# Halving the instructions that make the low parts of the second-layer weights, for all experts

## The chip, the cores and the metric

The kernel runs on one core of a Trainium2 chip. The metric is the device time of one execution in microseconds (us), lower being better. Engines are named as in the profile: PE is TensorE, DVE VectorE, ACT ScalarE, POOL GpSimd and SP SyncE.

## The reference

Three layers follow one another. Attention over a window of 128 positions gives x, 2304 rows of 512. Eight experts then share the rows: each takes the 288 rows that it likes best among those not yet taken, and sends them through two matrices. A dense layer of two matrices with a sigmoid gate ends it.

```python
def _moe_ref(x, w_gate, w1, w2):            # x (2304, 512), w1 (8, 512, 1024), w2 (8, 1024, 512)
    ...                                     # assigned[token] = expert, 288 tokens each, by sorted logits
    for e in range(E):
        mask = assigned == e
        h = np.maximum(x[mask] @ w1[e], 0.0)
        out[mask] = h @ w2[e]

def _moe2_ref(x, w_in, w_out):              # w_in (512, 2048), w_out (2048, 512)
    h = x @ w_in
    g = h * (1.0 / (1.0 + np.exp(-h)))
    return g @ w_out
```

## The kernel before, in words

The first 160 us or so are the attention, which also keeps the dense layer's weights in SBUF (res_h, res_l). Then the experts run in the order in which a ranking on the core names them, and each is followed by its share of the dense layer. STAGES lists the 16 stages: "A" is an expert's two layers, "M" the dense layer for a batch of rows (256, 256, 256 and 384, twice).

Each product is made of three: a value is kept as a high part, rounded to the matmul's input type, and a low part, the remainder. `product` multiplies high by high, high by low, low by high. For the experts' weights this splitting is done while the kernel runs. A tile of the first layer (wa) or of the second (wb) is 128x512. SP loads wb_raw (L1089), ACT rounds it to wb_h (L1385), and POOL subtracts, wb_l = wb_raw - wb_h, in `low_b` (L1156). wb_l lies over wb_raw. For wa the last step is DVE's, in `low_a` (L1647). Both rings have four tiles. Tile w belongs to expert w // 8, and f = w % 8.

An A stage runs the products a (first layer, f = 0 to 7, 12 matmuls each) and b (second layer, 12 matmuls each) in the order a0 a1 a2 b0 a3 b1 ... a7 b5 b6 b7. An M stage runs 16 of each in the same order. SLOTS is this list; every engine walks it, does its own part of each slot, and waits on semaphores for the others. SPLIT_B says in which slot a tile of wb is split: tiles 0 to 3 of an expert near the end of the M stage before it, one to each a slot; tile f from 4 on in slot b of f - 2.

In M stages POOL also makes the low part of the hidden values, h_l (L1168), issues the gather of the next expert's rows (L1130) and the scatter of finished ones (L1144). In A stages DVE makes h_l (L1712).

DVE and PE rank the tokens for the next expert meanwhile, in short steps at fixed slots (HOOK_AT). DVE compares all keys with 91 thresholds (`test`, L1492, 128x1820), PE counts them in 20 small matmuls (L1192), DVE finds what was reached (L1516), PE sums it (L1196), DVE updates `base` (L1521) and starts the next test. PE's steps stand in order between the products: in an A stage step 0 follows b2, step 1 follows a5, step 2 follows b4, step 3 follows a7 and step 4 follows b7. DVE's part after step 3 is a test. Expert 7's A stage has no such steps.

PE waits for wb_l once ahead of each product b (L1279, in `expert_b`), not once for each half. In the first expert, w < FT1 = 8, `low_b` has two instructions of 256 columns to each tile.

Of the kernel before, what the change touches and what calls it, by code (L numbers as in the profile page):

```python
# [16 lines left out]
DM = H * D  # L17
# [9 lines left out]
FT1, FT2 = F1 // P, F2 // P  # L27
# [903 lines left out]
def experts(nc, w1, w2, x_dram, out, keep):  # L931
# [4 lines left out]
    with ExitStack() as ctx:  # L936
# [6 lines left out]
        def sem(name):  # L943
            return ctx.enter_context(nc.semaphore(name))
# [84 lines left out]
        wb_high, wb_low = sem("wb_high"), sem("wb_low")  # L1029
# [20 lines left out]
        def h_cols(s, f):  # L1050

            width = CAP if STAGES[s][0] == "A" else BATCH[STAGES[s][1]][1]
            return slice(COLS * (f % 3), COLS * (f % 3) + width)
# [15 lines left out]
        @block.sync  # L1069
        def _(sp):  # L1070
            expert = []
            for kind, w in LOADS:
                j, f = divmod(w, FT1)
                if j == len(expert):
                    sp.wait_ge(id_known, j + 1)
                    expert.append(sp.value_load(ids[0:1, j:j + 1], min_val=0, max_val=E - 1))
                e = expert[j]
                if (kind, w) == LOADS[4]:
                    sp.wait_ge(fetch_sent, 1)
                if kind == "a":  # L1080
                    if w >= RING:
                        sp.wait_ge(a_done, A_NO[tile_stage(w - RING)])
                    sp.dma_start(wa_raw[w % RING][:].rearrange("p (c m) -> p c m", c=DC),
                                 w1[bass.ds(e, 1), :, P * f:P * (f + 1)].rearrange("o (c p) m -> p (o c) m", p=P)
                                 ).then_inc(wa_loaded[w % RING], 16)
                else:
                    if w >= RING:
                        sp.wait_ge(b_done, B_NO[tile_stage(w - RING)])
                    sp.dma_start(wb_raw[w % RING][:],  # L1089
                                 w2[bass.ds(e, 1), P * f:P * (f + 1), :].rearrange("o p m -> (o p) m")  # L1090
                                 ).then_inc(wb_loaded[w % RING], 16)
            sp.wait_ge(scattered, 16 * TILES_OUT[-1])

        @block.gpsimd
        def _(pool):
            pool.memset(ones[:], 1.0).then_inc(ones_ready, 1)

            def thresholds(j):

                for n, step in enumerate(STEPS[j][0:HIGH_ROUNDS]):  # L1100
                    pool.iota(rungs[j][:, n, :], pattern=[[step, KW[j]]], base=0, channel_multiplier=0,
                              allow_small_or_imprecise_dtypes=True).then_inc(rungs_ready, 1)

            thresholds(0)
            pool.memset(test[:, KW[0] * AHEAD:SECOND], 0.0).then_inc(rungs_ready, 1)
            pool.memset(test[:, SECOND + KW[0] * (NT - AHEAD):SECOND + KW[0] * (NT - AHEAD - 1) + P], 0.0
                        ).then_inc(rungs_ready, 1)
            pool.iota(iota_row[:], pattern=[[1, BLOCK]], base=0, channel_multiplier=0,
                      allow_small_or_imprecise_dtypes=True).then_inc(init_seq, 1)
            pool.iota(part_no[:], pattern=[[0, 1]], base=0, channel_multiplier=1,  # L1110
                      allow_small_or_imprecise_dtypes=True).then_inc(init_seq, 1)

            pool.iota(tile_base[:].rearrange("p (b t) -> p b t", b=B), pattern=[[S // 64, B], [P // 64, TB]], base=0,
                      channel_multiplier=0, allow_small_or_imprecise_dtypes=True).then_inc(init_seq, 1)
            pool.wait_ge(ones_ready, 1)
            pool.affine_select(out=before[:], in_=ones[:], compare_op=ALU.is_gt, fill=0.0, base=0,
                               pattern=[[1, P]], channel_multiplier=-1).then_inc(init_done, 1)
            thresholds(1)
            pool.memset(test[:, KW[1] * NT:KW[1] * (NT - 1) + P], 0.0).then_inc(rungs_ready, 1)

            def fetch(j):

                pool.wait_ge(tokens_known, GR * (j + 1))
                if j >= 1:
                    pool.wait_ge(xt_done, DC * j)
                else:
                    for stored in keep["x_stored"]:
                        pool.wait_ge(stored, 2 * 16 * B)
                for a in range(GR):
                    pool.indirect_dma_start(  # L1130
                        out=rows[:, a, :], out_offset=None, in_=x_dram,
                        in_offset=bass.IndirectOffsetOnAxis(ap=tokens[:, GR * j + a:GR * j + a + 1], axis=0)
                    ).then_inc(gathered[a], 16)

            def store(k):

                pool.wait_ge(out_known, k + 1)
                for t in range(BATCH[k][1] // P):
                    if t % 2 == 0:
                        pool.wait_ge(out_even, EVEN_OUT[k] + t // 2 + 1)  # L1140
                    else:
                        pool.wait_ge(out_odd, ODD_OUT[k] + t // 2 + 1)
                    n = TILES_OUT[k] + t
                    pool.indirect_dma_start(  # L1144
                        out=out, in_=out_rows[t], in_offset=None,
                        out_offset=bass.IndirectOffsetOnAxis(ap=out_tokens[:, n:n + 1], axis=0)
                    ).then_inc(scattered, 16)

            def low_b(w):

                pool.wait_ge(wb_high, w + 1)

                n = 2 if w < FT1 else 1
                for piece in range(n):
                    at = slice(DM // n * piece, DM // n * (piece + 1))
                    pool.tensor_tensor(wb_l[w % RING][:, at], wb_raw[w % RING][:, at], wb_h[w % RING][:, at].bitcast(FP32),  # L1156
                                       ALU.subtract).then_inc(wb_low, 1)

            fetch(0)
            pool.memset(mark[:], 0.0).then_inc(fetch_sent, 1)  # L1160
            for n, (s, kind, f) in enumerate(SLOTS):
                if n in STORE_AT:
                    store(STORE_AT[n])
                if kind == "a" and STAGES[s][0] == "M" and (s, f) != (len(STAGES) - 1, FT2 - 1):
                    g = FT2 * STAGES[s][1] + f
                    cols = h_cols(s, f)
                    pool.wait_ge(g_high, g + 1)
                    pool.tensor_tensor(h_l[:, cols], h_raw[:, cols], h_h[:, cols].bitcast(FP32), ALU.subtract  # L1168
                                       ).then_inc(g_low, 1)
                for w in SPLIT_B.get(n, []):  # L1170
                    low_b(w)
                if n in FETCH_AT:
                    fetch(FETCH_AT[n])
            store(len(BATCH) - 1)

        @block.tensor
        def _(pe):
# [60 lines left out]
            def product(out_, weights_h, weights_l, cols_h, cols_l, start, stop):  # L1238

                nc.tensor.matmul(out_, weights_h, cols_h, start=start, stop=False)  # L1240
                nc.tensor.matmul(out_, weights_h, cols_l, start=False, stop=False)  # L1241
                return nc.tensor.matmul(out_, weights_l, cols_h, start=False, stop=stop)  # L1242
# [32 lines left out]
            def expert_b(s, i, f):  # L1275

                w = FT1 * i + f
                pe.wait_ge(relu_low, w + 1)
                pe.wait_ge(wb_low, w + 1 + min(w + 1, FT1))  # L1279
                if f == 0 and i >= 1:  # L1280
                    pe.wait_ge(out_even, EVEN_OUT[i])
                    pe.wait_ge(out_odd, ODD_OUT[i])
                for c in range(DC):
                    m = slice(P * c, P * (c + 1))
                    last = product(acc[c][:, 0:CAP], wb_h[w % RING][:, m], wb_l[w % RING][:, m],
                                   h_h[:, h_cols(s, f)], h_l[:, h_cols(s, f)], f == 0, f == FT1 - 1)
                    if f == FT1 - 1 and c < DC - 1:
                        last.then_inc(acc_done, 1)
                last.then_inc(b_done, 1)
# [465 lines left out]
```

## Time and profile before

| | |
|---|---|
| median of 3 runs | 849.39 us (848.35 to 851.86) |
| profiled execution, its own time | 851.72 us |
| its span | 849.7 us |
| PE busy | 823.1 us, 97% |
| DVE busy | 485.2 us, 57% |
| ACT busy | 331.4 us, 39% |
| POOL busy | 305.5 us, 36% |
| wb_l on POOL (L1156) | 72 instructions, 87.2 us |

A busy time is the sum over an engine's instructions, overlaps counted once. The span is shorter than the execution's own time by what lies ahead of the first and behind the last instruction. In the timeline a row has an instruction's start and duration in us, engine, line, operation, what it writes and reads, and in brackets the idle time before it and what ended that.

### The profile page before, as it was taken

The page shows a single profiled execution, that of the slowest core. Times are in us where ns is not written, and L with a number is a line of the kernel's source. Part 1 is how long each engine was busy: PE and PEld are TensorE (multiplying, and loading weights), DVE is VectorE, ACT ScalarE, POOL GpSimd, SP SyncE. Part 2 cuts the span into 40 slices and gives each one's busy share as a digit, 9 for nine tenths or more (in the row PEclk, how much of TensorE's full clock was granted, in tenths as well). Part 3 has the DMA queues.
Part 4 walks back from the last instruction along what each step waited for, and adds up shares of the span by engine and source line. Part 5 has one row for each costly group of instructions (what it writes and reads, how often), then busy time and mean ns, then how long its engine had stood idle before and what let it go on. Part 6 is the DMA issues. An engine that isn't in the chain of part 4 may idle for free.

```text
span 849.7 us, 17963 instructions
## 1 busy us (share of the span) xinstructions
PE 823.1 (97%) x6903; PEld 746.8 (88%) x6903; DVE 485.2 (57%) x1562; ACT 331.4 (39%) x767; POOL 305.5 (36%) x343
## 2 busy tenths in 40 slices
PE   9999999649999999999999999999999999999997
PEld 7888888539989998998899889988998999899996
DVE  6778777666654756566565343846665475542111
ACT  4666666304224333432433224333332433343221
POOL 1013447714336234333622244234323623433222
PEclk9999999858999999999999999999999999999999
DMA  9789987324022304300340031204302230430000
GB/s 132 128 179 197 175 177 211 102 84 130 14 74 65 114 1 128 101 26 14 115 125 2 8 120 59 78 2 128 113 14 68 71 115 1 128 99 26 1 1 37
DMA packets 149764, 71.43 MB, mean 84 GB/s; under 512 B 98736, under 2 KB 136112, under 8 KB 149680
## 3 DMA queue, kind: packets, MB, share of 16 engines
q1 hardware_dynamic: 144336, 60.56, 28.7%
q0 software_dynamic: 2976, 9.44, 3.5%
q8 instruction: 55, 0.90, 0.5%
q10 hardware_dynamic: 2368, 0.30, 0.3%
q14 instruction: 29, 0.24, 0.1%
HBM read 60.83 MB, written 9.44 MB: 83 GB/s over the span
## 4 chain that ended last, share of the span: by engine, by line
PE 73%; DVE 4%; DMA 1%; issue 1%; POOL 1%; ACT 0%; SPq 0%; POOLq 0%; DVEq 0%; ACTq 0%
PE hp L1240 12%; PE hp L1241 11%; PE hp L1242 11%; PE acc L1325 8%; PE acc L1327 8%; PE acc L1326 8%; PE acc L1240 4%; PE acc L1242 3%; PE acc L1241 3%; PE rt L1192 2%; DVE wa_l L1647 1%; DMA wa_raw<-in_moe_w_dram 1%; DVE test L1492 1%; DMA x_rows_sb<-x_rows,tokens 1%; PE rt L1207 1%
## 5 line engine op out<-in xcount | busy, mean ns | idle before, releaser
L1168 POOL TENSOR_TENSOR h_l<-h_raw,h_h 128x256 fp32r<-128x256 f32 (+1 forms) x127 | 114.7, 903 | 260.8 <-ACT h_h L1449 260.7
L1718 DVE TENSOR_TENSOR h_raw<-hp,gate 128x256 f32<-128x256 f32 (+1 forms) x128 | 58.5, 457 | 179.7 <-ACT gate L1441 178.2
L1240 PE MATMUL hp<-xy_h,res_h 128*128 128x256 f32 (+1 forms) x512 | 154.0, 301 | 0.0
L1241 PE MATMUL hp<-xy_l,res_h 128*128 128x256 f32 (+1 forms) x512 | 151.4, 296 | 0.0
L1242 PE MATMUL hp<-xy_h,res_l 128*128 128x256 f32 (+1 forms) x512 | 151.2, 295 | 0.0
L1156 POOL TENSOR_TENSOR wb_l<-wb_raw,wb_h 128x512 fp32r<-128x512 f32 (+1 forms) x72 | 87.2, 1216 | 129.0 <-ACT wb_h L1385 129.0
L1441 ACT ACTIVATE gate<-hp 128x256 f32<-128x256 f32 (+1 forms) x128 | 52.7, 412 | 195.4 <-PE hp L1242 181.0
L1325 PE MATMUL acc<-res_h,h_h 128*128 128x512 f32 x288 | 116.6, 405 | 0.0
L1327 PE MATMUL acc<-res_h,h_l 128*128 128x512 f32 x288 | 113.6, 394 | 0.0
L1326 PE MATMUL acc<-res_l,h_h 128*128 128x512 f32 x288 | 113.5, 394 | 0.0
L1240 PEld LDWEIGHTS hp<-xy_h,res_h 128*128 128x128 f32 x512 | 96.5, 188 | 3.6
L1241 PEld LDWEIGHTS hp<-xy_l,res_h 128*128 128x128 f32 x512 | 96.4, 188 | 3.4
L1242 PEld LDWEIGHTS hp<-xy_h,res_l 128*128 128x128 f32 x512 | 96.5, 188 | 0.0
L1449 ACT ACTIVATE h_h<-h_raw 128x256 fp32r<-128x256 f32 (+1 forms) x128 | 56.6, 442 | 68.9 <-DVE h_raw L1718 68.9
L1240 PE MATMUL acc<-h_h,wb_h 128*128 128x288 f32 x256 | 76.5, 299 | 0.0
L1240 PE MATMUL hp<-xy_h,wa_h 128*128 128x288 f32 x252 | 75.6, 300 | 0.0
L1242 PE MATMUL acc<-h_h,wb_l 128*128 128x288 f32 x256 | 75.2, 294 | 0.0
L1241 PE MATMUL acc<-h_l,wb_h 128*128 128x288 f32 x256 | 75.2, 294 | 0.0
L1241 PE MATMUL hp<-xy_l,wa_h 128*128 128x288 f32 x252 | 74.5, 296 | 0.0
L1242 PE MATMUL hp<-xy_h,wa_l 128*128 128x288 f32 x252 | 74.4, 295 | 0.0
L537 PE MATMUL o_ps<-v_rows,pT 128*128 128x65 f32 x576 | 71.5, 269 | 0.0
L537 PEld LDWEIGHTS o_ps<-v_rows,pT 128*128 128x128 f32 x576 | 69.4, 192 | 0.0
(236 smaller groups left out, 1679.7 us busy)
## 6 DMA issues: line engine op xcount, KB each, us to landing
wa_raw<-in_moe_w_dram SPq DMA_DIRECT2D x64, 256.0 KB, 3.4
wb_raw<-in_moe_w_dram SPq DMA_DIRECT2D x64, 256.0 KB
k_rows<-in_k_dram SPq DMA_DIRECT2D x64, 72.0 KB, 3.4
q_rows<-in_q_dram SPq DMA_DIRECT2D x60, 72.0 KB, 2.5
v_rows<-in_v_dram SPq DMA_DIRECT2D x32, 128.0 KB, 4.3
x_rows<-x_rows_sb SPq DMA_DIRECT2D x8, 512.0 KB, 3.3
stage<-in_moe_w_in_dram SPq DMA_DIRECT2D x8, 512.0 KB, 4.7
stage<-in_moe_w_out_dram SPq DMA_DIRECT2D x8, 512.0 KB, 3.7
```

What stands on the lines that cost most here:

```text
L537: last = nc.tensor.matmul(o_ps[s % 2][:, o:o + D + 1], weights, v_rows[g % RING_IN][:, kt, h, :], start=(i == 0), stop=(i == len(blocks) - 1))
L1156: pool.tensor_tensor(wb_l[w % RING][:, at], wb_raw[w % RING][:, at], wb_h[w % RING][:, at].bitcast(FP32), ALU.subtract).then_inc(wb_low, 1)
L1168: pool.tensor_tensor(h_l[:, cols], h_raw[:, cols], h_h[:, cols].bitcast(FP32), ALU.subtract).then_inc(g_low, 1)
L1240: nc.tensor.matmul(out_, weights_h, cols_h, start=start, stop=False)
L1241: nc.tensor.matmul(out_, weights_h, cols_l, start=False, stop=False)
L1242: return nc.tensor.matmul(out_, weights_l, cols_h, start=False, stop=stop)
L1325: nc.tensor.matmul(acc[t][:], h_h[:, m], res_h[:, o:o + DM], start=(b == 0), stop=False)
L1326: nc.tensor.matmul(acc[t][:], h_h[:, m], res_l[:, o:o + DM], start=False, stop=False)
L1327: last = nc.tensor.matmul(acc[t][:], h_l[:, m], res_h[:, o:o + DM], start=False, stop=(b == FT2 - 1))
L1441: nc.scalar.activation(gate[:, 0:width], hp[(A_NO[s, f] - 1) % 2][:, 0:width], ACT.Sigmoid).then_inc(sig_done, 1)
L1449: nc.scalar.activation(h_h[:, h_cols(s, f)], h_raw[:, h_cols(s, f)], ACT.Copy).then_inc(g_high, 1)
L1718: nc.vector.tensor_tensor(h_raw[:, h_cols(s, f)], hp[(A_NO[s, f] - 1) % 2][:, 0:width], gate[:, 0:width], ALU.mult).then_inc(g_done, 1)
```

## The change

`low_b` now makes two instructions of 256 columns for every tile, each of which raises the semaphore wb_low by one, and `expert_b` waits for twice the number of tiles. Nothing else is touched.

```diff
                 pool.wait_ge(wb_high, w + 1)
 
-                n = 2 if w < FT1 else 1
-                for piece in range(n):
-                    at = slice(DM // n * piece, DM // n * (piece + 1))
+                for piece in range(2):
+                    at = slice(DM // 2 * piece, DM // 2 * (piece + 1))
                     pool.tensor_tensor(wb_l[w % RING][:, at], wb_raw[w % RING][:, at], wb_h[w % RING][:, at].bitcast(FP32),
                                        ALU.subtract).then_inc(wb_low, 1)
...
                 pe.wait_ge(relu_low, w + 1)
-                pe.wait_ge(wb_low, w + 1 + min(w + 1, FT1))
+                pe.wait_ge(wb_low, 2 * (w + 1))
```

## Rows read from the trace of the kernel before

**Rows 1.** The page: busy time of TensorE, and its granted clock in 40 slices.
```profile
PE 823.1 (97%) x6903; PEld 746.8 (88%) x6903; DVE 485.2 (57%) x1562; ACT 331.4 (39%) x767; POOL 305.5 (36%) x343
...
PEclk9999999858999999999999999999999999999999
```
**Rows 2.** All waits of TensorE, 285 to 845 us: total, times, longest.
```profile
PE rt L1196 <- DVE reached L1516: 0.9, 2, 0.8
```
**Rows 3.** Groups by form: the whole-tile instructions (count, busy, mean ns, idle before).
```profile
L1156 POOL TENSOR_TENSOR wb_l<-wb_raw,wb_h 128x512 fp32r<-128x512 f32 x56 | 73.2, 1307 | 111.6 <-ACT wb_h L1385 111.6
```
**Rows 4.** Timeline, halves and DVE in the first expert; last row: L61 alone.
```profile
198.04 1.43 POOL L1156 TENSOR_TENSOR wb_l<-wb_raw,wb_h 128x256 fp32r<-128x256 f32 x2 [8.75 <-ACT wb_h L1385]
...
205.43 0.73 POOL L1156 TENSOR_TENSOR wb_l<-wb_raw,wb_h 128x256 fp32r<-128x256 f32 x1 [0.53 <-ACT wb_h L1385]
205.46 0.88 DVE L61 TENSOR_TENSOR liked<-liked,best 128x160 f32<-128x160 f32 x1
206.12 0.82 POOL L1156 TENSOR_TENSOR wb_l<-wb_raw,wb_h 128x256 fp32r<-128x256 f32 x1
...
208.25 2.11 DVE L1492 SCALAR_TENSOR_TENSOR test<-rungs,base,key_hi 128x1820 bf16<-128x1820 f32 x1
208.59 2.37 POOL L1156 TENSOR_TENSOR wb_l<-wb_raw,wb_h 128x256 fp32r<-128x256 f32 x1 [1.65 <-ACT wb_h L1385]
210.28 1.22 DVE L1647 TENSOR_TENSOR wa_l<-wa_raw,wa_h 128x512 fp32r<-128x512 f32 x1
210.91 1.19 POOL L1156 TENSOR_TENSOR wb_l<-wb_raw,wb_h 128x256 fp32r<-128x256 f32 x1
...
357.17 0.32 DVE L61 TENSOR_TENSOR liked<-liked,best 128x160 f32<-128x160 f32 x1
```
**Rows 5.** Timeline, expert 1: tiles 5 and 7, the last test, products b5 and b7.
```profile
289.10 1.32 POOL L1156 TENSOR_TENSOR wb_l<-wb_raw,wb_h 128x512 fp32r<-128x512 f32 x1 [1.97 <-ACT wb_h L1385]
...
295.03 0.38 PE L1240 MATMUL acc<-h_h,wb_h 128*128 128x288 f32 x1
...
296.19 1.33 POOL L1156 TENSOR_TENSOR wb_l<-wb_raw,wb_h 128x512 fp32r<-128x512 f32 x1 [2.50 <-ACT wb_h L1385]
296.39 3.04 DVE L1492 SCALAR_TENSOR_TENSOR test<-rungs,base,key_hi 128x1820 bf16<-128x1820 f32 x1
298.28 0.29 PE L1240 MATMUL acc<-h_h,wb_h 128*128 128x288 f32 x1
```
**Rows 6.** Timeline, expert 6: tile 7 and the start of b7.
```profile
699.72 1.32 POOL L1156 TENSOR_TENSOR wb_l<-wb_raw,wb_h 128x512 fp32r<-128x512 f32 x1 [2.48 <-ACT wb_h L1385]
...
701.80 0.29 PE L1240 MATMUL acc<-h_h,wb_h 128*128 128x288 f32 x1
```
**Rows 7.** Timeline, expert 7: tile 7 and the start of b7.
```profile
774.71 1.30 POOL L1156 TENSOR_TENSOR wb_l<-wb_raw,wb_h 128x512 fp32r<-128x512 f32 x1 [1.90 <-ACT wb_h L1385]
776.66 0.29 PE L1240 MATMUL acc<-h_h,wb_h 128*128 128x288 f32 x1
```
**Rows 8.** Timeline, the end of the first M stage: a tile and the next h_l.
```profile
262.01 1.30 POOL L1156 TENSOR_TENSOR wb_l<-wb_raw,wb_h 128x512 fp32r<-128x512 f32 x1
264.06 0.73 POOL L1168 TENSOR_TENSOR h_l<-h_raw,h_h 128x256 fp32r<-128x256 f32 x1 [0.75 <-ACT h_h L1449]
```
**Rows 9.** Timeline: expert 2 ahead of TensorE's wait, and its two waits.
```profile
361.83 1.28 POOL L1156 TENSOR_TENSOR wb_l<-wb_raw,wb_h 128x512 fp32r<-128x512 f32 x1 [9.65 <-ACT wb_h L1385]
361.87 1.79 DVE L1647 TENSOR_TENSOR wa_l<-wa_raw,wa_h 128x512 fp32r<-128x512 f32 x1
...
364.75 0.18 PE L1196 MATMUL rt<-reached,ones 128*128 128x8 bf16 x1 [0.76 <-DVE reached L1516]
...
539.24 0.18 PE L1196 MATMUL rt<-reached,ones 128*128 128x8 bf16 x1 [0.16 <-DVE reached L1516]
```
**Rows 10.** Windows: stretch, busy time of PE, PEld, DVE, ACT, POOL, granted clock, DMA.
```profile
170.00:175.00 5.00, 1.79 (x42) 1.45 (x42) 3.38 (x14) 0.00 (x0) 0.00 (x0) 0.50 0.00 0
...
353.00:377.00 24.00, 23.24 (x216) 22.72 (x215) 18.08 (x34) 8.02 (x18) 5.17 (x4) 1.00 0.31 94
```

## The prediction

> **What bounds the kernel now.** I read the page's busy times first, then the waits, then the timeline of each engine in one expert after another. TensorE is busy 97% of the span at full granted clock from the experts on [rows 1], and between 285 and 845 us it waited for anything only twice, 0.9 us in all [rows 2]. So the kernel is one long row of TensorE instructions, and the change can cost or give time in two ways alone: by making TensorE wait where it doesn't now, or by removing one of those two waits. POOL has time to spare (36% busy), so the longer work on it counts for nothing as a sum; what counts is when a tile of wb_l is complete, and when VectorE (DVE) gets its turn beside POOL.
>
> **What is added.** 56 whole-tile instructions (experts 1 to 7, eight tiles each) of 1.31 us [rows 3] become 112 halves. A half alone takes 0.73 us, and a pair that nothing disturbs 1.43 us (the second is recorded from 0.69 us after the first and lasts 0.73) [rows 4], so each tile is 0.12 us later and POOL has 56 x 0.12 = 7 us more work, off the path. The first expert's pairs stay. TensorE's wait is now for twice the tile number, as many as POOL signals, so it releases at the second half of the same tile; it gains nothing from the first half, since its one wait stands ahead of the whole tile.
>
> **What the halves do to DVE's turn.** DVE and POOL exclude each other in some instructions. DVE's test, which compares 128x1820 values, takes 2.11 us alone [rows 4], but 3.04 us where it starts 0.20 us after a whole wb_l [rows 5]: it ends 1.91 us after POOL's instruction (299.43 against 297.52), as if it had waited for that one's end. The other way round, a half that POOL started at 208.59, inside a test that ended at 210.36, ended at 210.96, 0.60 us after the test [rows 4]. Who is next after a half, with a DVE instruction waiting and POOL's second half behind? The first expert shows it. The mask of `liked` (L61) started at 205.46, 0.03 us behind a half, and ended at 206.34; alone it takes 0.32. The second half, recorded from 206.12, ended at 206.94, which is 0.60 after L61's end. With POOL's second half first, L61 would have ended no earlier than 206.9. Likewise wa_l at 210.28 waited for the half that ended at 210.96 and ended at 211.50, and the next half, from 210.91, ended at 212.10, again 0.60 us behind [rows 4]. So DVE slips in between two halves. With a whole tile it can't.
>
> The Trainium skill, "SBUF — State Buffer", section "Who interferes with whom", says that a DVE instruction with two SBUF inputs and a GpSimd instruction that reads SBUF share a port pair as an exclusive lock held for the whole instruction. The 3.04 us agree. The same page gives about 115 ns from DVE's end to the blocked side's start for a transfer's descriptors; with a half of 0.73 behind it the second half would end 0.85 us after the test and the sum below would be 1.5 us higher, by that estimate. The measured 0.60 decides.
>
> **Where that meets TensorE.** Take the last tile (f = 7) of expert 1 [rows 5]. Now: wb_l starts at 296.19, is complete at 297.52, and TensorE starts its product (b of f = 7) at 298.28, without waiting: slack 0.76 us. DVE's test of the next ranking starts at 296.39. After the change, on the same clock: first half ends at 296.19 + 0.73 = 296.92; the test goes next and ends at 296.92 + 1.91 = 298.83; the second half ends at 298.83 + 0.60 = 299.43; a semaphore takes some 0.05 us to TensorE, so the product starts at 299.48 and not at 298.28. Stall: 1.20 us. Ahead of it TensorE has nothing else to do, since its stream is in order; behind it stands everything, the 20 small ranking products, the rest of the stage, the next.
>
> The order repeats, for both instructions hang on the same h_h of ScalarE: in experts 1 to 6 the last wb_l starts at 296.19, 373.07, 449.41, 547.54, 623.86 and 699.72, the test 0.19 or 0.20 us later, and the product 2.08 or 2.09 us after wb_l (the first is shown in [rows 5], the last in [rows 6]). Six stalls x 1.20 = 7.2 us.
>
> **Where it doesn't.** Tile f = 5 meets a test in five experts too (wb_l at 289.10 in expert 1), and would be complete at 289.10 + 0.73 + 1.91 + 0.60 = 292.34; its product starts at 295.03 [rows 5]: 2.7 us of cover, and if that were gone it would cost as much again as f = 7. In expert 2 it is only the one-column `base` that it meets. In expert 7 there is no ranking left: the last tile, 774.71 + 1.43 = 776.14, is still ahead of 776.66 [rows 7]. Tiles 0 to 3 are split in the dense stage behind a h_l; POOL is idle 0.75 us before the next h_l [rows 8], and a pair takes 0.12 more. Even with a DVE instruction between, the product that takes that h_l stands two products behind. Cost: 0; in the worst case 0.1 us x 28 = 3 us. SyncE's loads hang on TensorE's b_done and shift with it.
>
> **What is gained.** TensorE's two waits, 0.76 us at 364.75 and 0.16 us at 539.24, end at DVE's reached, which is late behind wa_l. In expert 2 wa_l started at 361.87, 0.04 us behind a whole wb_l, and took 1.79 us [rows 9]. By the first expert's pattern [rows 4] it takes 1.22, ending at 363.10 and not 363.66, and the second half ends at 363.10 + 0.60 = 363.70. The next wa_l, which would start at 363.39, waits for that and ends 0.54 later (as 211.50 stands to 210.96), at 364.24, not at 363.95 + 0.67 = 364.62: 0.4 us. In expert 4 the 0.16 us go whole. Sum of gains 0.56 us; bounds -0.9 (both waits vanish) and +0.3 (each wa_l sees 0.13 us more).
>
> **Sum.** 7.2 - 0.56 = +6.6 us: the profiled execution of 851.72 us (span 849.7 and 2.0 around it) would become 858.3. It was the high end of the three runs; from their median of 849.39 the same +6.6 gives 856.0. About 0.5%, 4.2 us, can be told from no change here; the forecast is 0.8%. Its own range: a stall of 0.9 to 1.5 us (each of the three terms, 0.73, 1.91 and 0.60, off by 0.1), gains 0 to 0.9: +4.5 to +9, so 853.9 to 858.4.
>
> **Rivals.** (A) POOL keeps the turn for its second half. Then the last tile is complete at P + 1.43, against the product at P + 2.09 (P: wb_l's start), so no stall, and DVE is 0.12 us later: the two waits grow to at most 1.2 us. Time 849.7. For it: halves are issued back to back in undisturbed pairs. Against it: the three places in [rows 4], all with DVE between; though none of these has a test waiting, only shorter instructions. Chance 0.14.
> (B) The other side: DVE's earlier turn is all that matters, because the second half still comes by P + 2.03. Place: the two waits of [rows 9]; price -0.9 us at most, plus run-to-run drift; it decides if a test between halves delays the second by less than 0.6 us instead of 2 us. That would need them to overlap, against the 2.37 us half of [rows 4]. Time 848.5. Chance 0.05.
> (C) The stalls do more: the granted clock falls after them. It stood at 0.50 (1.2 of 2.4 GHz) where TensorE was 36% busy [rows 10], but stayed at 1.00 through the 0.76 us wait of expert 2 [rows 10], and the new waits are 1.2 us. If half a microsecond more went after each, or the dense stage's 3 us came on top, it would be 859 to 861. Chance 0.06.
> Forecast: 0.75.
>
> The range of 849.0 to 860.0 holds the forecast, most of C and the upper part of A. Faster by over 0.5%: 0.02 (no mechanism reaches it, only drift on top of B); within 0.5%: 0.20 (A, the rest of B, and 0.03 from the weak end of the forecast); slower: 0.78 (the rest of the forecast and C).
>
> **What would show it.** In the waits, TensorE on wb_l of POOL: six times, about 1.2 us each, 7 us in all, in experts 1 to 6 and none in 7. In the timeline, the last tile's halves 0.73 us and about 2.5 us long, and the test between them 2.45 us, not 3.04. The clock stays at 1.00. The wait of expert 2 shrinks to about 0.4 us. Wrong, if the test ends after both halves (A), if the second half ends while the test runs (B), or if TensorE starts the last product within 0.2 us of where it does now.

## The result, and the profile after

| | before | after |
|---|---|---|
| median, 8 runs each | 849.62 us (847.55 to 854.01) | 855.74 us (855.21 to 858.5) |
| profiled execution, its own time | 851.72 us | 855.71 us |
| its span | 849.7 us | 853.8 us |

The changed kernel is slower: ratio 1.0074, 95% interval 1.0057 to 1.0091, so 6.3 us, between 4.8 and 7.7. Two executions at a lower granted clock are in no ratio: one of the kernel before (999.26 us, clock 0.746), timed beside the first four experiments, and one of their "A wait for each half" (900.66 us, 0.842). Each experiment's ratio is against the kernel before, timed beside it (medians 850.1, 849.87 and 849.61 us).

TensorE's waits from 285 us on (total, times, longest), against [rows 2]:

```profile
PE acc L1239 <- POOL wb_l L1155: 7.0, 6, 1.2
```

A wait that didn't exist before, six times, and the two waits for reached are gone. On the page POOL is busier and the clock is as before, against [rows 1]:

```profile
PE 822.1 (96%) x6903; PEld 744.5 (87%) x6903; DVE 478.8 (56%) x1562; ACT 331.4 (39%) x767; POOL 337.7 (40%) x399
...
PEclk9999999859999999999999999999999999999999
...
L1155 POOL TENSOR_TENSOR wb_l<-wb_raw,wb_h 128x256 fp32r<-128x256 f32 x128 | 119.3, 953 | 108.0 <-ACT wb_h L1384 107.9
```

POOL is busy 32 us longer, which is 25 us more than the 7 us that 56 instruction starts cost alone: the rest is halves that stand waiting for DVE, since a blocked instruction counts as busy. POOL's total says nothing of the cost; TensorE's waits do. Note also that DVE's busy time fell by 6 us, with the same instructions, in a slower kernel.

Now the last tile of expert 1, on POOL, DVE and TensorE, against [rows 5]. A timeline merges neighbours of one kind, so the pair appears as one row (x2), and its first half alone in a narrower window:

```profile
293.17 3.27 POOL L1155 TENSOR_TENSOR wb_l<-wb_raw,wb_h 128x256 fp32r<-128x256 f32 x2 [2.36 <-ACT wb_h L1384]
...
293.17 0.77 POOL L1155 TENSOR_TENSOR wb_l<-wb_raw,wb_h 128x256 fp32r<-128x256 f32 x1 [2.36 <-ACT wb_h L1384]
...
293.91 2.53 POOL L1155 TENSOR_TENSOR wb_l<-wb_raw,wb_h 128x256 fp32r<-128x256 f32 x1
...
293.37 2.48 DVE L1491 SCALAR_TENSOR_TENSOR test<-rungs,base,key_hi 128x1820 bf16<-128x1820 f32 x1
...
292.01 0.38 PE L1239 MATMUL acc<-h_h,wb_h 128*128 128x288 f32 x1
...
296.58 0.37 PE L1239 MATMUL acc<-h_h,wb_h 128*128 128x288 f32 x1 [1.17 <-POOL wb_l L1155]
```

The first half ends at 293.94, the test at 295.85 (1.91 later), the second half at 296.44 (0.58 to 0.59 later), the product b7 starts at 296.58 (0.15 later). Before, b7 started 3.25 us after b5 (295.03 to 298.28 in [rows 5]); now it is 4.57 us (292.01 to 296.58). So b7 starts 1.32 us late, 0.15 more than the 1.17 that the row calls idle: TensorE's matmuls overlap (one every 0.13 us, each recorded as 0.29 long), and the idle time is counted from the modelled end of the last one. Another 0.08 us goes behind the wait: b7's first matmul is recorded as 0.37 us long and the second starts at 296.79, 0.21 us after it, where before they started about 0.13 us apart (298.28 and 298.40). A stall costs 1.4 us in all. Expert 6 is the same, against [rows 6]:

```profile
702.37 3.27 POOL L1155 TENSOR_TENSOR wb_l<-wb_raw,wb_h 128x256 fp32r<-128x256 f32 x2 [2.33 <-ACT wb_h L1384]
702.57 2.48 DVE L1491 SCALAR_TENSOR_TENSOR test<-rungs,base,key_hi 128x1820 bf16<-128x1820 f32 x1
705.78 0.37 PE L1239 MATMUL acc<-h_h,wb_h 128*128 128x288 f32 x1 [1.17 <-POOL wb_l L1155]
```

In expert 7, where no test runs, the pair is undisturbed and b7, which begins at 780.74, doesn't wait, as in [rows 7]:

```profile
778.78 1.43 POOL L1155 TENSOR_TENSOR wb_l<-wb_raw,wb_h 128x256 fp32r<-128x256 f32 x2 [1.75 <-ACT wb_h L1384]
```

Where the time went, by the start of each expert's first product b (us from the span's start):

| expert | before | after | after minus before | growth over the expert ahead |
|---|---|---|---|---|
| 1 | 277.75 | 274.75 | -3.00 | |
| 2 | 353.75 | 352.14 | -1.61 | +1.39 |
| 3 | 430.98 | 429.76 | -1.22 | +0.39 |
| 4 | 528.84 | 529.02 | +0.18 | +1.40 |
| 5 | 605.44 | 606.65 | +1.21 | +1.03 |
| 6 | 681.39 | 684.04 | +2.65 | +1.44 |
| 7 | 757.61 | 761.68 | +4.07 | +1.42 |

Each row adds one stall of about 1.4 us, less in two of them where a wait of before went, and from expert 7 on nothing is added (92.09 us to the end of the span before, 92.12 after). The experts' part grew by 7.07 us. The profiled execution of before had come to them 3 us later than that of after: its first product of all started at 193.76 us with 1.76 us of waiting for gathered rows just before, against 192.71 us, and its granted clock was 0.95 between 195 and 226 us, against 1.00 (over its first 6.9 us of products 0.68, against 1.00 over the first 4.9 us after). The whole 3 us are there at the first expert's own first product b, 200.54 against 197.52 us. That is run-to-run drift ahead of the edited code, and it explains why the two spans differ by 4.1 us and not by 7.

### The profile page after: what moved, and what is told of

The parts are those of the page before. It is cut to its first block, busy times and chain, and to the rows that moved or that the text cites. A ratio compares the mean times of both kernels' runs of the same rounds, so it can differ in the third digit from the quotient of the medians.

```text
span 853.8 us, 18019 instructions
## 1 busy us (share of the span) xinstructions
PE 822.1 (96%) x6903; PEld 744.5 (87%) x6903; DVE 478.8 (56%) x1562; ACT 331.4 (39%) x767; POOL 337.7 (40%) x399
## 4 chain that ended last, share of the span: by engine, by line
PE 73%; POOL 3%; DVE 2%; ACT 1%; issue 1%; DMA 0%; POOLq 0%; DVEq 0%; ACTq 0%
PE hp L1239 12%; PE hp L1240 12%; PE hp L1241 12%; PE acc L1324 8%; PE acc L1326 8%; PE acc L1325 8%; PE acc L1239 3%; PE acc L1241 3%; PE acc L1240 3%; POOL wb_l L1155 2%; PE rt L1191 2%; PE rt L1206 0%; DVE test L1487 0%; PE acc L1233 0%; ACT wb_h L1384 0%
## 5 line engine op out<-in xcount | busy, mean ns | idle before, releaser
L1155 POOL TENSOR_TENSOR wb_l<-wb_raw,wb_h 128x256 fp32r<-128x256 f32 x128 | 119.3, 953 | 108.0 <-ACT wb_h L1384 107.9
```

## The experiments

Theory: a half lets DVE's test in ahead of the second half, which then waits for all of it, and the last tile of experts 1 to 6 has no slack for that. Each `PARTS[w]` below is the number of instructions for tile w, with TensorE's wait adapted to their sum.

**Only the last tile in halves.**

```diff
-                for piece in range(2):
+                for piece in range(PARTS[w]):
...
+PARTS = [2 if w < FT1 or w % FT1 == FT1 - 1 else 1 for w in range(E * FT1)]
```

> Halves only for the last tile (f = 7) of experts 1 to 7, and for the first expert as before; all other tiles whole. Theory (DVE's test slips in between the halves of the last tile): six waits of TensorE on wb_l of 1.16 us, so about +7 us against the kernel before, 856 to 857 us: all of the change's cost with 7 of its 56 added instructions. Rival (the 56 added instructions cost about evenly, as work of POOL or as delay of DVE in many places): 7 of 56 of 6 us, under +1 us.

Measured: 857.69 us, 0.7 above the range expected, ratio 1.0103 (1.0077 to 1.0129). Seven of the added instructions give the whole cost, and the rival's "under 1 us" is out. TensorE's waits from 275 to 785 us:

```profile
PE acc L1240 <- POOL wb_l L1156: 7.0, 6, 1.2
PE rt L1196 <- DVE reached L1516: 0.9, 1, 0.9
```

The new wait is the same; one wait for reached is back, in expert 2, whose tile 4 is whole here.

**All but the last tile in halves.**

```diff
+PARTS = [2 if w < FT1 or w % FT1 < FT1 - 1 else 1 for w in range(E * FT1)]
```

> Halves for all tiles but the last (f = 7) of experts 1 to 7, which stay whole: 49 of the 56 added instructions. Theory: no wait of TensorE on wb_l, within 1 us of the kernel before (849 to 850 us). Rival (added instructions cost evenly): +5 us.

Measured: 849.37 us, ratio 0.9986 (0.9972 to 1.0000). No wait on wb_l; one for reached of 0.34 us, in expert 5. The other 49 instructions, and the tests that split some of their tiles, cost nothing that can be measured.

**The test one slot later.**

```diff
-for _n in ((9, 10, 13, 14) if _j == 1 else (8, 9, 12, 13))
+for _n in ((9, 10, 13, 14) if _j == 1 else (8, 9, 12, 14))
```

> All tiles in halves, but step 3 of the ranking stands one slot later in experts 1 to 6 (behind b5 and not ahead of it), so DVE's test comes 1.6 us later, when the second half has started. Theory: the pair ends 1.43 us after its start, the test behind it at +3.3 us, and TensorE's waits on wb_l vanish; 849.5 to 850.5 us. Rival (the halves' later end alone, without the test, makes TensorE wait, or two signals cost): 855 to 856 us as with the change.

Measured: 848.82 us, ratio 0.9985 (0.9966 to 1.0005). Every tile is still in halves, and TensorE waits on none; it waits once for reached, 0.35 us in expert 5. POOL and DVE at the last tile of expert 1:

```profile
293.03 1.43 POOL L1155 TENSOR_TENSOR wb_l<-wb_raw,wb_h 128x256 fp32r<-128x256 f32 x2 [2.36 <-ACT wb_h L1384]
...
293.83 0.64 DVE L1520 SCALAR_TENSOR_TENSOR base<-digit,base 128x1 f32<-128x1 f32 x1
294.51 2.12 DVE L1491 SCALAR_TENSOR_TENSOR test<-rungs,base,key_hi 128x1820 bf16<-128x1820 f32 x1
```

Both run at their undisturbed length. `base`, one column wide, now meets the second half (0.64 us, not 0.16), and so holds the test back until POOL is done. So it is not the halves and not the second signal: it is the test between them.

**A wait for each half.**

```diff
-                pe.wait_ge(wb_low, 2 * (w + 1))
...
                 for c in range(DC):
+                    if c % 2 == 0:
+                        pe.wait_ge(wb_low, 2 * w + 1 + c // 2)
```

> All tiles in halves, and TensorE waits for the first half ahead of the product's first two column blocks and for the second half ahead of the third. Theory: b7 starts where it did before, runs 6 of its 12 matmuls (0.79 us) and then waits for the second half: 1.17 - 0.79 = 0.38 us six times, 2.3 us instead of 7.0, so 4.7 us less than the changed kernel, about 851 us. Rival (a wait ahead of the third block costs by itself, 64 times): no gain over the changed kernel, 855 us or more.

Measured: 852.72 us (852.61 without the execution at the lower clock), ratio 1.0031 (1.0014 to 1.0048), 3 us under the changed kernel's median, where 4.7 were expected. The wait moves behind six matmuls and shrinks from 1.17 to 0.30 us:

```profile
PE acc L1239 <- POOL wb_l L1155: 1.8, 6, 0.3
```

In the last tile of expert 1:

```profile
294.43 3.27 POOL L1155 TENSOR_TENSOR wb_l<-wb_raw,wb_h 128x256 fp32r<-128x256 f32 x2 [2.36 <-ACT wb_h L1385]
...
297.76 0.40 PE L1239 MATMUL acc<-h_h,wb_h 128*128 128x288 f32 x1 [0.30 <-POOL wb_l L1155]
```

I expected 0.38. The idle time reads low again: the matmul at 297.76 starts 0.59 us after the one ahead of it and the next 0.24 after that, both 0.13 undisturbed, so a stall costs 0.57 us. From expert 1's first product b to expert 7's the trace is 5.0 us shorter than the changed kernel's (481.89 against 486.93), which is six times the difference of 1.41 and 0.57; that the medians are only 3 us apart was not traced, but executions of one kernel spread by as much. The last tile's stall is a matter of when its second half is there.

**The test in two instructions.**

```diff
-                nc.vector.scalar_tensor_tensor(at_least, rung[:, None, :].to_broadcast([P, NT, k]),
+                for tiles in (slice(0, NT // 2), slice(NT // 2, NT)):
+                    last = nc.vector.scalar_tensor_tensor(at_least[:, tiles], ...
...
+                last.then_inc(dve_part, 1)
```

> The changed kernel, with DVE's test made by two instructions of 10 token tiles each, for experts 1 to 6's rankings (the wb_l tiles stay in halves). Theory (each side gets its turn when the other's instruction ends): POOL's second half waits for the first part of the test alone, about 0.95 us less, so TensorE's wait on wb_l falls from 1.17 to about 0.2 to 0.3 us six times; 850.5 to 852 us. Rival (once DVE has the turn it keeps it for all that it has queued): the waits stay at 1.2 us or grow by the second instruction's start, 856 to 857 us.

Measured: 851.96 us, ratio 1.0026 (1.0006 to 1.0047); six waits of 0.23 us on wb_l. They aren't all that this version pays: TensorE's wait for a test in the first expert is 0.86 us and not 0.24, and in expert 5 it waits 0.23 us for a h_l. In the last tile of expert 1:

```profile
293.37 2.33 POOL L1155 TENSOR_TENSOR wb_l<-wb_raw,wb_h 128x256 fp32r<-128x256 f32 x2 [2.36 <-ACT wb_h L1384]
...
293.56 1.53 DVE L1492 SCALAR_TENSOR_TENSOR test<-rungs,base,key_hi 128x910 bf16<-128x910 f32 x1
...
293.56 3.10 DVE L1492 SCALAR_TENSOR_TENSOR test<-rungs,base,key_hi 128x910 bf16<-128x910 f32 x2
```

First half to 294.14, first part of the test to 295.09, second half to 295.70 (0.6 behind it), second part of the test to 296.66 (0.96 behind that). The two engines take turns, instruction by instruction. The rival, DVE keeping the turn while it has more queued, is out.

**The last tile in four parts.**

```diff
+PARTS = [4 if w >= FT1 and w % FT1 == FT1 - 1 else 2 for w in range(E * FT1)]
```

> The last tile (f = 7) of experts 1 to 7 in four parts of 128 columns, all others in halves as in the changed kernel. Theory (one gap behind the first part lets the test in; after it nothing of DVE's is queued that excludes POOL): the first part ends some 0.3 us earlier and the test with it, but three parts come behind it and not one; in all two more instruction starts of 0.12 to 0.15 us, waits of 1.4 to 1.5 us, 857 to 858 us. Rival (a shorter first instruction shortens the wait, since the test starts earlier): waits under 1.0 us, 854 to 855 us.

Measured: 858.16 us, ratio 1.0095 (1.0065 to 1.0124); TensorE's waits from 275 to 785 us:

```profile
PE acc L1240 <- POOL wb_l L1156: 8.7, 6, 1.4
```

The timeline of the test and the tile in expert 1:

```profile
294.96 2.21 DVE L1492 SCALAR_TENSOR_TENSOR test<-rungs,base,key_hi 128x1820 bf16<-128x1820 f32 x1
...
294.76 3.54 POOL L1156 TENSOR_TENSOR wb_l<-wb_raw,wb_h 128x128 fp32r<-128x128 f32 x4 [2.36 <-ACT wb_h L1385]
```

The finer the pieces, the sooner DVE gets in (the test takes 2.21 us, barely blocked) and the later the tile is complete (3.54 us): 1.45 us of waiting instead of 1.17.

**Whole tiles everywhere, the first expert too.**

```diff
+PARTS = [1] * (E * FT1)
```

> All tiles whole, in the first expert too. Theory: there the halves let DVE in sooner (its wa_l took 1.22 and 0.85 us beside them), so TensorE's wait for reached, 0.37 us at 213.14 in the kernel before, grows by 0.3 to 0.7 us, and no wait on wb_l appears, since the first expert's last tile meets no test. Rival (the halves never helped there): the wait stays at 0.4 us.

One execution, 852.04 us, which tells little: its first product of the experts started at 196.26 us, 2.5 us later than the profile of before, ahead of the edited code. TensorE's wait for reached in the first expert, and what DVE did ahead of it:

```profile
210.83 1.77 DVE L1647 TENSOR_TENSOR wa_l<-wa_raw,wa_h 128x512 fp32r<-128x512 f32 x1
...
212.90 1.40 DVE L1647 TENSOR_TENSOR wa_l<-wa_raw,wa_h 128x512 fp32r<-128x512 f32 x1
...
214.79 0.18 PE L1196 MATMUL rt<-reached,ones 128*128 128x8 bf16 x1 [1.47 <-DVE reached L1516]
```

The two wa_l take 3.17 us, where they took 1.22 and 0.85 beside halves in the kernel before (the first is in [rows 4]). TensorE waits 1.47 us, not 0.37; I had expected 0.3 to 0.7 more and it is 1.1. From the first expert's first product b to the next expert's it is 78.34 us, against 77.21 before. In the first expert halves pay, because there DVE is late and wb_l is not. Between 275 and 785 us this run had no wait at all, the two of [rows 9] included, though its tiles were whole.

**Whole tiles with the test one slot later.**

> The kernel before (whole tiles in experts 1 to 7) with step 3 of the ranking one slot later, as in the run e3_test_later. Theory: it had no wait on wb_l to lose, so the place of the step is worth nothing by itself: within 1 us of the kernel before, the waits for reached as there; the 1 us that e3_test_later lies below the kernel before comes from the halves. Rival (the later step is what gains): 848 to 849 us here too.

The edit is that of the third experiment on the kernel before. Measured: 848.80 us, ratio 0.9997 (0.9983 to 1.0012), one wait for reached of 0.54 us. The median is the one that the rival names, the ratio shows no gain, so the times don't tell the two apart; the traces do, under "The gains" below.

**Both: all but the last tile in halves, and the test later.**

> Halves for all tiles but the last of experts 1 to 7 (as in e2_all_but_last), and step 3 of the ranking one slot later (as in e3_test_later). Theory: neither a wait on wb_l nor, but for a late load, one for reached; what can still be had is the 1 us that those waits cost in the kernel before, so 848 to 849.5 us, 0 to 0.2% below it, at the edge of what five rounds can tell. Rival (the two edits gain by different means and add up): 2.5 us below the kernel before.

Measured: 848.84 us, ratio 0.9997 (0.9981 to 1.0013), with no wait for wb_l or reached between 275 and 785 us. The two edits' effects don't add up, and no version beats the kernel before by more than can be told.

## Why the prediction was right

**The turn between two halves.** Forecast from three places of the first expert; shown by the turns of the halved test, by the test's 2.48 us (2.45 forecast) and by the second half's end 0.59 us behind it (0.60).

**The place.** Six stalls, in experts 1 to 6, at the last tile, none in 7, none at tile 5. Halving that tile alone brings the whole cost, all others none, and moving the test by a slot takes it away with all halves in place.

**The size of a stall.** Forecast 1.20 us in b7's start, measured 1.32. The first half took 0.77, not 0.73, because `base` runs beside it (DVE, 293.18 to 293.34); with `base` later, in the third experiment, it took 0.73. From POOL's end to TensorE's start it was 0.15 us, where I had taken 0.05 for a semaphore. The 0.08 us behind the wait was in no term. Six stalls: 6 x 1.4 = 8.5 us with the growth of the table's undisturbed rows (1.39 to 1.44, mean 1.41), not 7.2.

**The gains.** Forecast 0.56 us, measured 1.4. The ranking step between a5 and b3 came 2.58 us and 1.99 us after a5 had started (362.17 to 364.75, 537.25 to 539.24) where 1.68 is undisturbed, so the two waits held it up by 0.90 and 0.31 us; in the table, where a row lacks 1.02 and 0.38 us of a stall, they cost 1.4. Both are gone.

In expert 2 most of this need not be the change's doing. There DVE was also late because a load of wa took 3.9 us (issued at 350.93, awaited until 354.81), against 3.0 us in the profile after (349.31 to 352.33). In whole-tile profiles the wait in expert 2 was 0.76, 0.89 and 0.54 us, and none in one; in the seven with tile 4 in halves it was never there, but two of those waited 0.34 and 0.35 us in expert 5. The wait in expert 2 goes with that load in every profile: ACT began to round it 1.06, 1.21 and 1.30 us after the expert's first product b in the three that waited, 0.41 us in the whole-tile one that didn't, and 0.07 to 0.25 us in the seven with halves. So those seven never met so late a load there; whether the halves have a part in that, no run shows.

In expert 5 that load's rounding began 1.20 and 1.09 us after in the two of the seven that waited for reached, so halved tiles don't do away with the wait. That halves shorten it is in the turns shown, and no run compares the two at one lateness. Where loads are prompt they gain nothing after the first expert: from expert 1's first product b to expert 7's it is 478.58 us with whole tiles everywhere and 478.46 us in the last experiment, both without a wait of TensorE.

**The sum.** 8.5 - 1.4 = 7.1 us, the table's 7.07, against 6.6 forecast: both terms were taken too low, and most of the two errors cancels out. That is in part luck, since the larger gain hangs on a late load in the profile of before: against whole tiles with prompt loads (478.58 us) the changed kernel's 486.93 is 8.4 us more. The timed difference is 6.1 us of the medians, and 6.3 (4.8 to 7.7) by the ratio.

**The rivals.** A (POOL keeps the turn) is out by every profile that has the last tile in pieces and the test beside it. B (only the freed waits matter) named a gain, of 1.4 us rather than 0.9 and not shown to be the halves' own, that the stalls outweigh. C: the granted clock stayed at 1.00 through the stalls, against [rows 10] (window, then busy time of PE, PEld, DVE, ACT and POOL, clock, DMA):

```profile
377.00:700.00 323.00, 319.50 (x2462) 294.02 (x2461) 176.17 (x466) 111.50 (x255) 137.50 (x147) 1.00 0.22 68
```

Two stretches beside it, 277 to 377 us and 700 to 785 us, show 1.00 too, and the dense stages cost nothing: against [rows 8], a pair there took 1.44 us and left POOL idle for 0.57 us, and TensorE didn't wait:

```profile
259.04 1.44 POOL L1155 TENSOR_TENSOR wb_l<-wb_raw,wb_h 128x256 fp32r<-128x256 f32 x2
261.05 0.73 POOL L1167 TENSOR_TENSOR h_l<-h_raw,h_h 128x256 fp32r<-128x256 f32 x1 [0.57 <-ACT h_h L1448]
```

The Trainium skill's 115 ns ("SBUF — State Buffer", "A bandwidth-pool intuition that's wrong (but worth ruling out)") are measured there on a transfer's descriptors and don't carry over: the second half's end, 0.59 us behind the test, is even less than its own 0.73 us. So some 0.14 us of the half's length overlap its wait; what the engine does in them, no run here shows. The prediction's other sentence on that page ("Who interferes with whom") holds here: the page says "for the whole instruction" of DVE's two-port modes, and the test, an instruction with two inputs in SBUF, kept POOL's half from ending until 0.59 us behind it.

## What to carry to other kernels

Where two engines exclude each other instruction by instruction, the size of an instruction is also the size of a turn. Splitting it helps the other engine and hurts its own result, which then waits for a whole instruction of the other: split where the neighbour is late, keep whole where the result is. Before splitting, look for the longest instruction that can fall into the gap and compare it with the slack of the consumer, here 2.1 us against 0.76 us; the same edit gains in the first expert and loses in six others.

## What the runs showed of the hardware that I had not expected

The exclusion takes instructions that are very small: `base`, one column of 128 rows, took 0.64 us behind half a tile and 1.16 us behind a whole one (365.17 us in the kernel before), against 0.16 us.

Where a product waits as a whole, TensorE starts about 0.15 us after POOL's instruction ends, and about 0.05 us after DVE's (reached, ended at 364.70, its matmul at 364.75 in [rows 9]). That is not a property of POOL: with a wait for each half, b7's third column block started 0.05 us after POOL's second half (294.43 + 3.27 = 297.70, to 297.76). What makes the other 0.1 us is open.
